# Linear attention rebuilt on channel-major r and k, halves of 64 tokens and 64x64 array tiles, ahead of a mixture of experts and a dense pair

## Chip, cores and metric

One core of one Trainium2 chip. The metric is the device time of one execution in microseconds (us). The profile follows one execution and shows five engines: PE (TensorE, with PEld for its weight loads), DVE (VectorE), ACT (ScalarE), POOL (GpSimd) and SP (SyncE, which here only issues DMAs).

## What is computed

```python
# stage 1: decaying linear attention; B=4, H=8 heads, S=768 tokens, D=48 channels
state = zeros(B, H, D, D)
for t in range(S):
    cur = einsum('bhd,bhe->bhde', u * k[t], v[t])
    y[t] = einsum('bhd,bhde->bhe', r[t], state + cur)
    state = w[:, :, None] * state + einsum('bhd,bhe->bhde', k[t], v[t])
x = y as rows of 384, one for each of the 3072 tokens
# stage 2: route every token to its best expert of 8
expert = argmax(x @ w_gate); gate = its softmax probability
x = gate * (relu(x @ w1[expert]) @ w2[expert])          # 384 -> 1024 -> 384
# stage 3: dense pair 384 -> 2048 -> 384
h = x @ w_in;  out = maximum(0.01 * h, h) @ w_out
```

All inputs are fp32.

## The kernel before

Stage 1 works in 24 units: 6 chunks of 128 tokens by 4 pairs of heads, each unit with all 4 batches. `rn`, `kn` and `vp` hold r, k and v with the 128 tokens on partitions and the two heads of a pair side by side (96 columns). In a unit:

- POOL multiplies k by u (L360), that by r (L363); DVE sums it to one number per token and head (L473, `own`); POOL multiplies v by it (L369). This is each token's own term of y.
- DVE scales r and k by powers of w (L475, L476).
- PE transposes both to channel-major (`transposes`, L721 and L723), ACT copies them out of PSUM (L653, and twice L655, once for each head with the other head's channels at zero).
- PE makes the scores k^T r of 128x128 tokens for each batch and head (L768), DVE masks them (L540), PE multiplies them with v into `ps_y` (L807).
- PE makes the unit's k^T v (L789) and r times the old state (L792); DVE adds the former to `state` and decays it (L549, L553), and adds the own term to `ps_y` into `yc` (L577).

A finished chunk is routed during the next: PE transposes its 4x3 blocks of `yc` (`tile`, L736), ACT copies them (L663), PE makes the logits (L746) and the ranks within experts (L753, L754). DVE runs 16 small steps (`routing`), ACT the exponential and the gating of rows (L669, L676), and POOL scatters the rows to their experts' places in DRAM (L384). POOL also splits the first expert's seven weight pieces into a high and a low part (`split_piece`, L133 and L137): four in chunk 1, two behind the last unit's work, one between the last two scatters. Chunks 1 to 4 stand in a hardware loop of two turns. Every engine has its own queue and order; they meet by semaphores. SP loads each unit's r, k and v with six DMAs.

Stages 2 and 3 come after a barrier. The edit changes nothing in them but the name of PSUM banks.

Of the kernel before, what the change touches and what calls it, by code (L numbers as in the profile page):

```python
# [6 lines left out]
I32 = mybir.dt.int32  # L7
# [6 lines left out]
def build_program(nc, r, k, v, w, u, moe_w_gate, moe_w1, moe_w2, moe2_w_in, moe2_w_out, out):  # L14
    P = 128
    B, H, S, DH = r.shape
    D = H * DH
    E = moe_w_gate.shape[1]
    FE = moe_w1.shape[2]
    FD = moe2_w_in.shape[1]  # L20
    C = S // P
    HP = H // 2
    W2 = 2 * DH
    N = B * S
# [7 lines left out]
    T0 = P // 2 + 1  # L32
# [17 lines left out]

    def att(a):
        return a.rearrange("b (q t) (c p) d -> c q t p b d", q=HP, p=P)

    r_v, k_v, v_v = att(r), att(k), att(v)
# [23 lines left out]
    with ctx:  # L78
# [8 lines left out]

        bank = [pb(f"bank{i}") for i in range(8)]
# [62 lines left out]
        with st1:  # L151
            rn = sb("rn", [P, HP, B, W2], stack=st1)
            kn = sb("kn", [P, HP, B, W2], stack=st1)
            vp = sb("vp", [P, HP, B, 2, W2], stack=st1)
            pr = sb("pr", [P, HP, B, W2], stack=st1)
            own = sb("own", [P, HP, B, 2], stack=st1)
            k_blk = sb("k_blk", [W2, B, 2, P], stack=st1)
            r_t = sb("r_t", [W2, 2, B, P], stack=st1)
            am = sb("am", [P, B, 2, P], stack=st1)
            state = sb("state", [W2, HP, B, W2], stack=st1)  # L160
            tab_r = sb("tab_r", [P, D], stack=st1)
            tab_k = sb("tab_k", [P, D], stack=st1)
            u_b = sb("u_b", [P, D], stack=st1)
            w_end = sb("w_end", [W2, HP, W2], stack=st1)
            yc = sb("yc", [P, 2, B, XW], stack=st1)
            x_t = sb("x_t", [P, 2, DC, P], stack=st1)
            wg = sb("wg", [P, DC, E], stack=st1)
            mask = sb("mask", [P, P], stack=st1)
            ones = sb("ones", [P, P], stack=st1)
            head = sb("head", [W2, 2], stack=st1)  # L170
            w_col = sb("w_col", [W2, 2, HP], stack=st1)
            pw = sb("pw", [W2, 2, HP, P + 2], stack=st1)
            warm = sb("warm", [W2, HP], stack=st1)
            w_128 = sb("w_128", [W2, HP], stack=st1)
            rank = sb("rank", [P, E], stack=st1)
            gate = sb("gate", [P, 2, B], stack=st1)
            tok_no = sb("tok_no", [P, 2, B], I32, stack=st1)

            mx = sb("mx", [P, B], stack=st1)
            sh = sb("sh", [P, B, E], stack=st1)  # L180
# [1080 lines left out]
```

## Time and profile before

| | |
|---|---|
| median of 3 runs | 875.04 us (869.81 to 875.75) |
| the profiled execution | 882.38 us, of it span 880.6 us |
| stage 1's units, first scores to last row | 17.27 to 203.97 us |
| granted TensorE clock, mean | 0.97 |

The profiled execution is 1.008 times the median. Times in the rows are from the start of its span. A matmul row gives how long one record takes through the array; records overlap, so their pace is read from the starts of runs of them. One fp32 product is two records (L768 has 384 for 24 units of 8 products), one transpose is one record.

### The profile page before, as it was taken

The numbers are of one execution on the slowest core, as the hardware profiler recorded it, in microseconds if no ns is written. First come the engines' busy times: TensorE is split into PE (matmuls) and PEld (weight loads), VectorE is DVE, ScalarE is ACT, GpSimd is POOL, SyncE is SP. The second block draws the span as 40 slices with busy tenths as digits, with TensorE's granted clock in tenths as the row PEclk, the third lists the DMA queues.
The fourth block names the chain that finished last, engine by engine and source line by source line (L and its number), as shares of the span: only waits on it lengthen the run. The fifth ranks groups of instructions, "written<-read, shape, count | busy, mean of one in ns | idle before, by whom it ended". The sixth has DMA issues, their size and how long they took to land.

```text
span 880.6 us, 13367 instructions
## 1 busy us (share of the span) xinstructions
PE 822.3 (93%) x4856; PEld 772.8 (88%) x4856; DVE 370.7 (42%) x711; ACT 227.2 (26%) x422; POOL 361.3 (41%) x383
## 2 busy tenths in 40 slices
PE   3999999995499999988998999999999999999996
PEld 3999899995499999988997998898998998998895
DVE  5766576865222333222226343243343343243222
ACT  1224233332111221211111323233223223223221
POOL 7684564474366778767989301001001001001001
PEclk9999799996699999999999999999999999999998
DMA  8679345421647655565444100000000000000000
GB/s 165 149 189 224 66 107 119 79 80 54 151 103 107 142 141 140 99 129 127 146 143 109 36 1 37 1 1 36 0 1 37 0 0 36 0 0 36 1 1 36
DMA packets 109523, 66.72 MB, mean 76 GB/s; under 512 B 85901, under 2 KB 103341, under 8 KB 109485
## 3 DMA queue, kind: packets, MB, share of 16 engines
q1 hardware_dynamic: 96008, 50.96, 26.1%
q10 hardware_dynamic: 10405, 5.79, 3.4%
q0 software_dynamic: 3072, 9.45, 2.8%
q8 instruction: 24, 0.39, 0.2%
q14 instruction: 14, 0.11, 0.0%
HBM read 51.62 MB, written 14.59 MB: 75 GB/s over the span
## 4 chain that ended last, share of the span: by engine, by line
PE 51%; POOL 14%; issue 5%; DMA 2%; DVE 1%; POOLq 0%; SPq 0%; ACT 0%; DVEq 0%
PE bank L1077 23%; PE bank L1056 23%; POOL w_lo L137 9%; POOL w_hi L133 4%; PE bank L1018 3%; DMA stage<-in_moe_w 2%; PE bank L1002 2%; POOL tick L123 1%; DVE x_hi L1197 0%; POOL out_rows L946 0%; DVE x_lo L1200 0%; PE bank L985 0%; POOLq L130 0%; POOLq L136 0%; SPq L897 0%
## 5 line engine op out<-in xcount | busy, mean ns | idle before, releaser
L946 POOL DMA_INDIRECT out_rows<-rows,ids_i x24 | 23.4, 974 | 359.6 <-ACT rows L1153 354.1
L1218 DVE TENSOR_TENSOR h_lo<-gf,h_hi 128x512 fp32r<-128x512 f32 x96 | 68.7, 716 | 228.3 <-ACT h_hi L1144 226.5
L137 POOL TENSOR_TENSOR w_lo<-stage,w_hi 128x768 fp32r<-128x768 f32 (+1 forms) x70 | 146.8, 2097 | 5.8
L1077 PE MATMUL bank<-w_hi,h_hi 128*128 128x384 f32 x384 | 130.4, 340 | 0.0
L1077 PE MATMUL bank<-w_lo,h_hi 128*128 128x384 f32 x384 | 129.3, 337 | 0.0
L1077 PE MATMUL bank<-w_hi,h_lo 128*128 128x384 f32 x384 | 129.1, 336 | 0.0
L1140 ACT ACTIVATE hc<-bank 128x512 f32<-128x512 f32 x96 | 57.5, 599 | 273.2 <-PE bank L1056 273.2
L1056 PE MATMUL bank<-x_hi,w_hi 128*128 128x512 f32 x288 | 114.0, 396 | 2.2 <-DVE x_lo L1200 2.2
L1056 PE MATMUL bank<-x_lo,w_hi 128*128 128x512 f32 x288 | 114.1, 396 | 0.0
L1056 PE MATMUL bank<-x_hi,w_lo 128*128 128x512 f32 x288 | 113.8, 395 | 0.0
L1182 DVE SCALAR_TENSOR_TENSOR h_lo<-bank,h_hi 128x416 fp32r<-128x416 f32 x64 | 37.9, 592 | 147.9 <-ACT h_hi L1121 147.9
L1077 PEld LDWEIGHTS bank<-w_hi,h_hi 128*128 128x128 f32 x384 | 72.1, 188 | 7.1 <-issue 3.5
L1121 ACT ACTIVATE h_hi<-bank 128x416 fp32r<-128x416 f32 x64 | 33.1, 517 | 172.7 <-PE bank L1002 172.7
L1077 PEld LDWEIGHTS bank<-w_hi,h_lo 128*128 128x128 f32 x384 | 72.2, 188 | 3.5
L133 POOL TENSOR_SCALAR w_hi<-stage 128x768 fp32r<-128x768 f32 (+1 forms) x70 | 65.2, 932 | 20.6 <-DMA stage<-in_moe_w 20.3
L1018 PE MATMUL bank<-h_hi,w_hi 128*128 128x416 f32 x192 | 67.9, 354 | 5.0 <-POOLq L143 5.0
L1077 PEld LDWEIGHTS bank<-w_lo,h_hi 128*128 128x128 f32 x384 | 72.2, 188 | 0.0
L1215 DVE SCALAR_TENSOR_TENSOR gf<-bank,hc 128x512 f32<-128x512 f32 x96 | 65.7, 684 | 12.1 <-ACT hc L1140 12.1
L1002 PE MATMUL bank<-x_hi,w_hi 128*128 128x416 f32 x192 | 67.8, 353 | 0.1
L1002 PE MATMUL bank<-x_lo,w_hi 128*128 128x416 f32 x192 | 67.5, 352 | 0.0
L1002 PE MATMUL bank<-x_hi,w_lo 128*128 128x416 f32 x192 | 67.5, 352 | 0.0
L1018 PE MATMUL bank<-h_hi,w_lo 128*128 128x416 f32 x192 | 67.2, 350 | 0.0
(148 smaller groups left out, 1387.3 us busy)
## 6 DMA issues: line engine op xcount, KB each, us to landing
stage<-in_moe_w SPq DMA_DIRECT2D x24, 512.0 KB, 5.9
stage<-in_moe_w SPq DMA_DIRECT2D x32, 384.0 KB, 3.2
rows<-x_rows ACTq DMA_DIRECT2D x9, 625.6 KB
x_rows<-pad_row SPq DMA_DIRECT2D x8, 625.6 KB
rn<-in_r SPq DMA_DIRECT2D x48, 96.0 KB, 2.6
kn<-in_k SPq DMA_DIRECT2D x48, 96.0 KB, 2.7
vp<-in_v SPq DMA_DIRECT2D x48, 96.0 KB, 2.6
stage<-in_moe_w_in SPq DMA_DIRECT2D x6, 512.0 KB, 3.9
```

The source lines that it names most:

```text
L133: eng.tensor_scalar(w_hi[:, buf, off:off + cols], stage[:, h, 0:cols], 1.0, 0.0, ALU.mult, ALU.add).then_inc(split_hi, 1)
L137: i = eng.tensor_tensor(w_lo[:, buf, off:off + cols], stage[:, h, 0:cols], w_hi[:, buf, off:off + cols].bitcast(F32), ALU.subtract)
L946: pool.indirect_dma_start(out, bass.IndirectOffsetOnAxis(ap=idx.bitcast(U32), axis=0), rows[:, t, 0:D], None).then_inc(stored, 16)
L1002: i = pe.matmul(ps_h[f % 2][:, 0:U], ww[:, b, o:o + P], x[:, b, d, 0:U], start=d == 0 and ww is w_hi and x is x_hi, stop=d == DC - 1 and x ...
L1018: i = pe.matmul(ps_y[d][:, 0:U], ww[:, b, o:o + P], h[:, f % NB, 0:U], start=f == 0 and ww is w_hi and h is h_hi, stop=f == FC - 1 and h i ...
L1056: i = pe.matmul(ps_h[f % 2][:, :], ww[:, 0, o:o + P], x[:, b, d, :], start=d == 0 and ww is w_hi and x is x_hi, stop=d == DC - 1 and x is ...
L1077: i = pe.matmul(ps_o[t][:, 0:D], x[:, f % NB, t * P:(t + 1) * P], ww[:, 1, o:o + D], start=f == 0 and x is h_hi and ww is w_hi, stop=f == ...
L1121: act.activation(h_hi[:, f % NB, 0:U], ps_h[f % 2][:, 0:U], ACT.Relu).then_inc(h_hi_ok, 1)
L1140: act.activation(hc[:, f % 2, :], ps_h[f % 2][:, :], ACT.Copy).then_inc(d_ok, 1)
L1182: dve.scalar_tensor_tensor(h_lo[:, f % NB, 0:U], ps_h[f % 2][:, 0:U], 0.0, h_hi[:, f % NB, 0:U].bitcast(F32), ALU.max, ALU.subtract).then_ ...
L1215: dve.scalar_tensor_tensor(gf[:, f % 2, :], ps_h[f % 2][:, :], 0.01, hc[:, f % 2, :], ALU.mult, ALU.max).then_inc(g_ok, 1)
L1218: dve.tensor_tensor(h_lo[:, f % NB, :], gf[:, f % 2, :], h_hi[:, f % NB, :].bitcast(F32), ALU.subtract).then_inc(gl_ok, 1)
```

## The change

- The host lays r and k out channel-major, v token-major with both heads side by side; SP loads a unit with four DMAs of 96 KB (2 KB runs) and one of 192 KB. Channels of the first head are on partitions 0 to 47, those of the second on 64 to 111; partitions between are zeroed once.
- The PE transposes of r and k, and the ACT copies of them, go. Instead PE transposes the scaled k alone to token-major (`k_rows`) and ACT copies it (`ka_copy`).
- A chunk of 128 tokens is taken as two halves of 64. Scores are made within a half only; the state is carried from half to half (`x_st`, four slots; `v_st`, the decayed copy made by ACT).
- The products address 64 rows by 64 columns of the array: scores, k^T v, r times state, and scores times v.
- The own term's sum over channels is a product with `sel` on PE (in `k_rows`) in place of the DVE reduction.
- DVE makes r*u*k in one instruction, and scales r; POOL scales k.
- `yc` has three buffers instead of two; the logits use two column halves of the array.
- All of stage 1 is written out, without loops; all seven splits of the first expert's weights lie in it.

The core of the diff (loads, dropped parts and the setup of tables left out):

```diff
             @blk.gpsimd
+                def scaled_k(g):
+                    pool.wait_ge(ruk_ok, g + 1)
+                    pool.tensor_tensor(kk, kk, pw[...], ALU.mult).then_inc(k_ok, 1)
+                def own_terms(g):
+                    pool.wait_ge(ka_out, g + 1)
+                    pool.tensor_tensor(pr[:, g % 2], v_u[:, i], a_s..., ALU.mult).then_inc(own_ok, 1)
+                scaled_k(0)
+                scaled_k(1)
+                pool.memset(tick[:, :], 0.0).then_inc(consts, 1)
+                pool.iota(...)                       # five of them, each .then_inc(consts, 1)
+                for g in range(UN):
+                    scaled_k(g + 2)
+                    own_terms(g + 1)
+                    if c >= 2 and q == 0:
+                        scatter(c - 2)
+                    if g in SPLIT_AT:                # {1: 0, 2: 1, 4: 2, 5: 3, 7: 4, 10: 5, 14: 6}
+                        split_piece(...)
             @blk.vector
+                def scale(g):
+                    dve.scalar_tensor_tensor(ruk[0:R2, g % 2], k_u[0:R2, i], u_col[0:R2, q:q + 1], r_u[0:R2, i],
+                                             ALU.mult, ALU.mult).then_inc(ruk_ok, 1)
+                    dve.tensor_tensor(rr, rr, pw[...], ALU.mult).then_inc(r_ok, 1)
+                def masks(g):
+                    dve.wait_ge(s_mm, g + 1)
+                    dve.tensor_tensor(am[:, g % 2], ps_s[...], mask_l[...], ALU.mult).then_inc(masked, 1)
+                def state(g, j):
+                    dve.wait_ge(m_mm, g + 1)
+                    dve.scalar_tensor_tensor(x_st[0:R2, q, slot(c, j + 1)], ps_m[0:R2, j, 0:B * DH], w_64[0:R2, q:q + 1],
+                                             v_st[0:R2, q], ALU.mult, ALU.add).then_inc(x_ok, 1)
+                for g in range(UN):
+                    masks(g + 1)
+                    scale(g + 2)
+                    # routing steps, if c > 0 and q >= 2
+                    state(g + 1, 0)
+                    rows_out(g)
+                    state(g + 1, 1)
             @blk.scalar
+                for g in range(UN):
+                    ka_copy(g + 1)                   # 128x448 and 128x8 out of PSUM
+                    # x_copy, exponentials
+                    decayed(g + 1, 0)
+                    # x_copy
+                    decayed(g + 1, 1)
+                    # gates
             @blk.tensor
+                def scores(g):
+                    pe.wait_ge(r_ok, g + 1)
+                    pe.wait_ge(k_ok, g + 1)
+                    for b in range(B):
+                        for j in range(2):
+                            for t in range(2):
+                                ins = pe.matmul(ps_s[halves[j], t, b * L:(b + 1) * L], k_u[heads[t], i, b, halves[j]],
+                                                r_u[heads[t], i, b, halves[j]], start=True, stop=True)
+                def k_rows(g):
+                    for b in range(B):
+                        pe.transpose(ps_x[:, b * R2:(b + 1) * R2], k_u[0:R2, i, b, :], ident[0:R2, 0:R2])
+                    for b in range(B):
+                        for j in range(2):
+                            ins = pe.matmul(ps_x[halves[j], KA + 2 * b:KA + 2 * b + 2], ruk[0:R2, g % 2, b, halves[j]],
+                                            sel[0:R2, :], start=True, stop=True)
+                def update(g):
+                    for b in range(B):
+                        for j in range(2 if c < C - 1 else 1):
+                            for t in range(2):
+                                ins = pe.matmul(ps_m[heads[t], j, b * DH:(b + 1) * DH],
+                                                km[halves[j], b, heads[t]], v_u[halves[j], i, t, b, :], ...)
+                def from_state(g):
+                    for b in range(B):
+                        for j in range(2):
+                            for t in range(2):
+                                pe.matmul(ps_y[halves[j], t, b * DH:(b + 1) * DH], r_u[heads[t], i, b, halves[j]],
+                                          x_st[heads[t], q, slot(c, j), b * DH:(b + 1) * DH], ...)
+                def within(g, other):
+                    for b in range(B):
+                        for j in range(2):
+                            t = 1 - j if other else j
+                            ins = pe.matmul(ps_y[halves[j], t, b * DH:(b + 1) * DH], am[halves[j], g % 2, t, b, :],
+                                            v_u[halves[j], i, t, b, :], ...)
                 def logits(c, b):
                     for d in range(DC):
-                        i = pe.matmul(ps_lg[:, b, :], x_t[:, b % 2, d, :], wg[:, d, :], ...)
+                        for j in range(2):
+                            ins = pe.matmul(ps_lg[halves[j], b, :], x_t[:, b, d, halves[j]], wg[:, d, :], ...)
+                pe.wait_ge(consts, CONSTS)           # 9
+                scores(0); k_rows(0); update(0)
+                for g in range(UN):
+                    scores(g + 1)
+                    # logits(c, 2 * q - 1) if 0 < q < 3
+                    k_rows(g + 1)
+                    from_state(g)
+                    within(g, False)
+                    update(g + 1)
+                    # tile(c, 2 * q) if q < 2; ranks if q == 2
+                    within(g, True)
+                    # logits(c, 2 * q), tile(c, 2 * q + 1) if q < 2
+                pe.wait_ge(y_out, UN)
+                for b, to in enumerate((ps_x, ps_s[:, 0], ps_m[:, 0], ps_s[:, 1])):
+                    tile(C, b, to)
```

## Rows read from the trace of the kernel before

**Rows 1.** The page: share of the span in which each engine is busy.
```profile
PE 822.3 (93%) x4856; PEld 772.8 (88%) x4856; DVE 370.7 (42%) x711; ACT 227.2 (26%) x422; POOL 361.3 (41%) x383
```

**Rows 2.** Stretches: length, busy PE, PEld, DVE, ACT, POOL; clock, DMA share, GB/s.
```profile
77.24:113.37 36.13, 33.82 (x266) 33.35 (x265) 19.93 (x50) 11.08 (x21) 17.97 (x22) 0.86 0.55 120
113.37:144.04 30.67, 29.37 (x267) 28.63 (x266) 23.44 (x50) 11.08 (x21) 18.06 (x22) 1.00 0.49 103
...
203.97:232.13 28.16, 7.82 (x41) 7.35 (x41) 8.41 (x51) 4.32 (x9) 10.31 (x10) 0.54 0.32 94
232.13:464.00 231.87, 226.69 (x1242) 224.08 (x1243) 65.28 (x111) 44.02 (x88) 175.43 (x172) 0.99 0.59 130
```

**Rows 3.** Timeline of PE, one unit without routing: start, duration, group, count.
```profile
25.48 1.98 PE L768 MATMUL bank<-r_t,k_blk 96*128 96x128 f32 x16
27.30 0.60 PE L721 MATMUL bank<-ident,rn 128*96 128x128 f32 x4
...
28.17 0.84 PE L789 MATMUL bank<-vp,kn 128*96 128x96 f32 x8
28.85 1.06 PE L792 MATMUL bank<-state,r_t 96*128 96x96 f32 x8
29.74 1.95 PE L807 MATMUL bank<-vp,am 128*128 128x96 f32 x16
31.53 1.98 PE L768 MATMUL bank<-r_t,k_blk 96*128 96x128 f32 x16
```

**Rows 4.** Timeline of PE behind a wait: the first two logit records together.
```profile
155.65 0.29 PE L746 MATMUL bank<-wg,x_t 128*128 128x8 f32 x2
```

**Rows 5.** The same two records by line: shortest, median, longest duration in ns.
```profile
L746 PE MATMUL bank<-wg,x_t x2: 175/216/256, 155.6 to 155.7; 128*128 128x8 f32 x2
```

**Rows 6.** DVE's groups in the units: count, busy us, mean ns, idle before.
```profile
L540 DVE TENSOR_TENSOR am<-bank,mask 128x512 f32<-128x512 f32 x48 | 31.0, 682 | 4.6 <-PE bank L768 4.5
L476 DVE TENSOR_TENSOR kn<-kn,tab_k 128x384 f32<-128x384 f32 x22 | 20.4, 926 | 0.0
...
L549 DVE TENSOR_TENSOR state<-bank,state 96x384 f32<-96x384 f32 x24 | 13.3, 554 | 34.3 <-PE bank L792 31.2 <-remote 3.1
```

**Rows 7.** DVE's group of 512 elements from two SBUF tiles, stage 3.
```profile
L1218 DVE TENSOR_TENSOR h_lo<-gf,h_hi 128x512 fp32r<-128x512 f32 x96 | 68.7, 716 | 228.3 <-ACT h_hi L1144 226.5 <-issue 1.8
```

**Rows 8.** POOL's groups in the units.
```profile
L369 POOL TENSOR_TENSOR pr<-vp,own 128x192 f32<-128x192 f32 x46 | 29.0, 651 | 15.4 <-DVE own L473 9.9 <-DMA x_rows<-yc,row_i 5.5
L363 POOL TENSOR_TENSOR pr<-pr,rn 128x384 f32<-128x384 f32 x22 | 24.4, 1110 | 1.7
...
L384 POOL DMA_INDIRECT x_rows<-yc,row_i x17 | 16.9, 996 | 10.8 <-DVE row_i L527 5.9 <-issue 4.7
```

**Rows 9.** ACT's group of 512 elements out of PSUM in the units.
```profile
L653 ACT ACTIVATE r_t<-bank 96x512 f32<-96x512 f32 x23 | 13.6, 591 | 50.5 <-PE bank L723 43.4 <-issue 7.1
```

**Rows 10.** Timeline around a split: POOL's and DVE's instructions side by side.
```profile
36.19 2.36 POOL L137 TENSOR_TENSOR w_lo<-stage,w_hi 128x1024 fp32r<-128x1024 f32 x1
36.62 2.33 DVE L553 TENSOR_TENSOR state<-state,w_end 96x384 f32<-96x384 f32 x1
```

**Rows 11.** Timeline of the start: SP's issues and POOL's first product.
```profile
0.81 0.91 SPq L266 DMA_DIRECT2D w_col<-in_w  x2
1.77 0.47 SPq L271 DMA_DIRECT2D rn<-in_r  x1
...
8.88 1.00 POOL L360 TENSOR_TENSOR pr<-kn,u_b 128x384 f32<-128x384 f32 x1 [1.60 <-DMA vp<-in_v]
```

**Rows 12.** Timeline of the tail: DVE's first routing step of the last chunk.
```profile
211.40 0.19 DVE L492 TENSOR_REDUCE mx<-bank 128x4 f32<-128x32 f32 x1 [7.42 <-PE bank L746]
```

**Rows 13.** Timeline of PE in chunk 2, where the clock falls.
```profile
91.86 0.89 PE L789 MATMUL bank<-vp,kn 128*96 128x96 f32 x8 [1.92 <-DVE yc L577]
...
94.78 3.71 PE L807 MATMUL bank<-vp,am 128*128 128x96 f32 x16
98.28 3.67 PE L768 MATMUL bank<-r_t,k_blk 96*128 96x128 f32 x16
```

More of the change, by code:

```diff
@@ L151, in build_program @@
         with st1:
[L152 to L160, printed above, removed]
@@ new lines, in _ @@
+                link(pool.memset(sel[heads[1], 1:2], 1.0))
+                link(pool.affine_select(out=mask[:, :], in_=ones[:, :], compare_op=ALU.is_gt, fill=0.0,
+                                        base=0, pattern=[[1, P]], channel_multiplier=-1))
+                for j in range(2):
+                    link(pool.tensor_copy(mask_l[halves[j], :], mask[halves[j], halves[j]]))
+                pool.memset(v_st[:, :, :], 0.0).then_inc(consts, 1)
+                pool.memset(x_st[:, :, 0, :], 0.0).then_inc(consts, 1)
@@ L405, in _ @@
-                pool.sem_inc(yc_free, 1)
-                pool.sem_inc(yc_free, 1)
-                pc = expert_pieces(0)
-                chunk(0, 0)
-                chunk(1, 1)
-                with pool.Fori(0, C // 2 - 1) as t:
-                    chunk(t * 2 + 2, 0)
-                    chunk(t * 2 + 3, 1)
-                own_terms(C - 1, HP - 1)
-                for n in range(HP, NPE - 1):
-                    split_piece(pool, n, n % 2, 0, pc[n], n in ENDS)
-                scatter(C - 2, C % 2)
@@ L598, in _ @@
-                for q in range(HP):
-                    unit(C - 1, q, (C - 1) % 2, True)
-                routing(C, (C - 1) % 2, range(1, RS + 1))
+                dve.wait_ge(rows_0, 32)
+                scale(0)
+                scale(1)
+                dve.wait_ge(consts, CONSTS)
+                masks(0)
+                state(0, 0)
+                dve.tensor_copy(rank[:, :], rank_no[:, :])
+                dve.tensor_copy(region[:, :], region_no[:, :])
+                link(dve.tensor_copy(run[:, 0, :], region_no[:, :]))
@@ L603, in _ @@
+                for b in (1, 3):
+                    dve.wait_ge(yt_mm, (C - 1) * B + (b + 1))
+                    dve.tensor_copy(x_t[:, b].rearrange("p c t -> p (c t)"), ps_s[:, b // 2, 0:D]).then_inc(yt_dve, 1)
+                routing(C, range(1, RS + 1))
                 dve.wait_ge(route, C * RS + RS)
@@ L745, in logits @@
                     for d in range(DC):
[L746 removed]
+                        for j in range(2):
+                            ins = pe.matmul(ps_lg[halves[j], b, :], x_t[:, b, d, halves[j]], wg[:, d, :],
+                                            start=d == 0, stop=d == DC - 1)
                     if b == B - 1:
[L748 removed]
+                        ins.then_inc(lg_mm, 1)
                 def ranks(c):
```

659 lines of the change are left out of this document (301 added, 358 removed).

## The prediction, made before the result was known

> **What bounds the kernel now.** I read the page first: PE is busy 93% of the span [rows 1]. An average over three stages says little, so I cut the span into stretches [rows 2]. Stages 2 and 3 (from 232.13 us) keep PE full and are not edited; what the change is worth must come out of the 232.13 us before them: start 17.27, units 186.70, tail 28.16. In the units PE is the bound: in a steady chunk of 30.67 us it is busy 29.37, DVE 23.44, POOL 18.06, ACT 11.08 [rows 2].
>
> The busy time of PE counts overlapping records, so I price by pace, from starts of successive runs [rows 3]. 16 records of L768 (128 stationary columns, 128 moving) fill 25.48 to 27.30, 0.114 us each; L807 (128 stationary, 96 moving) 0.112; L792 the same, 0.111; the transposes 0.109; L789 (96 stationary, 96 moving) 0.085. With 96 moving columns the pace still follows the stationary ones: 0.112 at 128, 0.085 at 96, so 0.00084 a column. A unit is 16 x 0.114 + 8 x 0.109 + 8 x 0.085 + 8 x 0.111 + 16 x 0.112 = 6.05 us, which is the distance of the two L768 runs. Routing of a chunk adds 12 transposes, 24 logit records and 4 rank records: 12 x 0.109 + 28 x 0.112 = 4.4. A chunk is then 28.6, and the steady one takes 30.67: 2.1 of waits, some 0.5 a unit. Chunk 2 takes 36.13 because the clock fell (mean 0.86).
>
> **The new work of PE, in records.** Scores 32 (64 stationary columns), transposes of k 4 (128), sums with `sel` 16 (64), `update` 32 (48 stationary), `from_state` 32 (64), `within` 32 (64): 148 where there were 56. The rows fix the price only from both sides.
>
> - *One after another.* Continuing the line of the two paces, 64 stationary columns cost 0.058 and 48 cost 0.045. Then a unit is 32 x 0.058 x 3 + 32 x 0.045 + 4 x 0.11 + 16 x 0.058 = 8.4 us: PE loses 2.3 us a unit.
> - *Side by side.* If different corners of the array load and multiply at once, what is left is the distance at which PE can start records. The smallest that the trace shows: two logit records take 0.29 together while the second takes 0.256, so they start 0.03 apart [rows 4, 5]. At 0.03 the four array-tile products cost 128 x 0.03 = 3.84. The `sel` sums use all rows and split the array only by columns; the trace has nothing like it, I take the middle, 0.044: 0.7. With the transposes 0.45: 5.0.
>
> I take side by side: in every product except `update` two neighbours lie in different row halves, and 0.03 is a distance seen in this trace, though only between two records whose weights could be loaded during a wait. That is the weakest step here. A change between 64-wide and full use of the array may have to empty it; the trace has none. The bounds are nothing and the part of a record that overlap hides now, 0.275 - 0.112 = 0.16; I take 0.08 for each of 5 changes a unit, 0.4. So a unit is 5.4. Routing: 12 transposes 1.3, 48 half-width logit records x 0.044 = 2.1, ranks 0.45, changes of mode 0.4: 4.3 a chunk. With the old 2.1 of waits a chunk is 4 x 5.4 + 4.3 + 2.1 = 28.0.
>
> The Trainium skill has a rule on each side. TensorEngine Tiling (Array Packing), section Performance Considerations, gives each matmul some 60 cycles whatever its columns, which is an estimated 0.025 us at 2.4 GHz and near the 0.03 of the rows. The Trainium skill's page TensorE: Matmul & The Clock Gate, section "Wait — 56ns, not 53.3ns?", has a case in which firmware decodes each matmul at some 62 ns; by that 148 records would be an estimated 9.2 us and the change a loss. No row here has such short records in a long run, so it is open which holds.
>
> **The other engines' new work per unit.** DVE: the r*u*k and the r product are 512 elements from two SBUF tiles, 0.716 each when POOL is quiet [rows 7]; the 384-element L476 takes 0.926 next to POOL [rows 6], so up to 1.2 each: 1.4 to 2.4, taken 2.0. One mask of 512 instead of two, 0.68. Two state steps of 192 elements, each above half of L549's 0.554 and below it: taken 0.35, 0.7. Row output 0.55, as L549. Routing: some 0.9 (16 short steps over four units). Sum 4.8. POOL: `scaled_k` 512/384 x 1.11 = 1.5, `own_terms` two times 0.65 = 1.3 [rows 8], scatter four times 1.0 a chunk, and seven splits of about 3: 2.8 + 1 + 0.9 = 4.7. ACT: the copy of 448 elements about 0.6 [rows 9], small ones, two decays, routing: under 3. All below 5.4 to 7, so hidden as long as PE needs that; what a quick PE would meet is below.
>
> The new waits: `scores(g + 1)` stands first in PE's order and waits for r_ok and k_ok. Behind it everything of PE is queued. The ring is scores (1.0 and 0.15 to the end), masks 0.68, r*u*k 1.0, `scaled_k` 1.5, and four hand-overs that I put at 0.1: 4.7 us a unit, less than PE's own. POOL's splits stand in this ring's path and hold DVE's two-input instructions: the decay of the state, 384 elements, took 2.33 beside a split of 2.36 [rows 10]. A split begins after `own_terms`, and at 7 us a unit it is over before the next r*u*k is asked for. At cost nothing go: the three ACT copies and the DVE reduction (their engines were idle behind PE), the loads (five DMAs instead of six a unit, ahead of use), the third `yc` buffer (it only removes a wait for scatters), and the program's greater length, unless fetching it stalls PE.
>
> **Start and tail.** SP issues six small loads at about 0.45 and then ten of 0.5 up to unit 1's k and r, with two DMAs of zeros between [rows 11]: 0.8 + 2.7 + 2.5 + 1.0 + 2.0 = 9.0, landing at some 12. PE waits for nine constants, which POOL makes behind `scaled_k(1)`: 12 + 0.8 + 1.4 + 0.6 = 14.8, against 17.27. Gain 2.4. The bounds are 0 and 4.5 (if only unit 0 were waited for). In the tail the last row is out at 203.97 and the first routing step starts at 211.40 [rows 12], 7.4 later; four transposes into four banks, copies by two engines and 48 records of logits at the low clock make it about 5: gain 2.5, bounds 1 and 4. The rest of the 28.16 (routing, slot tables, last scatters, barrier, first loads) stays.
>
> **The sum.** Chunk 0, without routing: 4 x 5.5 and 2 for the low clock of the start, 24. Five chunks of 28.0, less 0.5 for the halved `update` of the last chunk times four units: 138. Together 162 against 186.7: 24.7 less; chunk 2's fall of the clock (5.5 us over a steady chunk) is part of that. With 2.4 and 2.5 it is 29.6. From 882.4 that gives 852.8 in the profiled execution, and divided by 1.008, 846 for the median. The largest unknown, the mode changes, moves this by 0.4 x 24 = 10 either way; the pace of `sel` sums and logits between 0.03 and 0.058 by about 9: 825 to 866 for this case.
>
> **The rivals.**
>
> *Slower: the 64-wide products don't overlap.* Unit 8.4 + 0.4, routing 12 x 0.109 + 48 x 0.058 + 0.45 + 0.4 = 4.9; chunk 4 x 8.8 + 4.9 + 2.1 = 42.2; together 38 + 211 - 3 = 246, 59 more than before, less 4.9: +54, 929. It decides from a mean pace of 0.038 us for the 128 tile records of a unit (where PE's new sum passes the old). For it: 2.6 times the records, and every long run in the trace keeps at least 0.085. Against: the trace's pace follows the width of the weights, and neighbours here use different rows. A mean near 0.04 would leave the time where it is. (The 62 ns of the Trainium skill's page TensorE: Matmul & The Clock Gate, same section, would end in this rival, an estimated 0.8 us a unit later still.)
>
> *PE out of the way.* If tiles start closer than 0.03, DVE, POOL and the ring of 4.7 us bound: with splits and scatters in POOL's order about 5.6 a unit, 24 x 5.6 + 2 = 136, 51 less, with start and tail 56 less: 820. For it: 4 corners at once would need only a quarter of 0.058.
>
> *The clock.* It fell in chunk 2 some 1.3 us after PE had waited 1.92, and L807 went from 0.112 to 0.219 a record [rows 13]. If small tiles with short waits keep the granted clock at its lower level, 1.2 GHz, for half of the units, PE adds some 5 a unit there, 60 in all, against the 30 gained: 905. For it: PE waits more where others catch up; against: most of the time PE stays the busiest.
>
> **Chances.** Forecast 0.45; PE out of the way 0.2; no overlap 0.2; low clock or overlap that is only partial, from 866 to 905, 0.15. The range for 8 in 10 goes from 815 to 915. A measurement of this kernel can't tell less than 1% from nothing. Faster by over 1% (below 866): 0.68; within 1% (866 to 884): 0.07; slower by over 1%: 0.25.
>
> **What will show it.** Starts of successive records of scores and `within`: 0.03 apart (forecast), near 0.058 (no overlap), under 0.02 (PE out of the way). Distance of two units' score runs: 5.5 without routing, 7 with. First scores at 14.8. The granted clock of the units near 0.95. DVE's mask waits for PE, not PE for k_ok. Wrong would make me: firmware-like pace of records, stalls of PE's fetch, mode changes that cost more than 0.16, or splits that hold the ring.

## The result, and the profile after

The changed kernel takes 885.45 us (883.44 to 886.74, 4 runs) where the kernel before takes 874.76 (869.81 to 875.75, 4 runs): ratio 1.013, 95% interval 1.009 to 1.018. It is slower by a little over 1%, where 846 was forecast. Medians here and below are of all executions, ratios only of those within 1.5% of their kernel's fastest. Its profiled execution took 883.44, with a span of 881.7.

The page, those lines of it that answer to [rows 1], and those in 40 slices that show the finding at once:

```profile
PE 816.5 (93%) x7136; PEld 752.5 (85%) x7136; DVE 336.8 (38%) x659; ACT 214.6 (24%) x435; POOL 334.3 (38%) x330
...
PEclk9875566555599999999999999999999999999999
```

PE's share is what it was, so the first line says nothing. The second does: a slice is 22 us, and from the fourth to the eleventh the granted clock is 0.5 to 0.6. The stretches, as in [rows 2] (length, busy PE, PEld, DVE, ACT, POOL; clock, DMA share, GB/s). From the row at 71.10 on, three rows hold four units each; the one before them holds three, the one behind them the last five:

```profile
0.00:18.28 18.28, 0.00 (x0) 0.00 (x0) 6.16 (x25) 1.50 (x3) 7.55 (x24) 1.00 0.60 134
18.28:47.94 29.66, 26.91 (x673) 24.69 (x673) 16.05 (x32) 6.70 (x18) 17.51 (x13) 0.85 0.78 205
47.94:71.10 23.16, 21.59 (x517) 18.88 (x515) 13.15 (x25) 6.65 (x18) 13.40 (x10) 0.72 0.78 230
71.10:105.68 34.58, 33.42 (x663) 29.48 (x661) 17.84 (x41) 9.62 (x25) 19.14 (x16) 0.50 0.49 142
105.68:139.65 33.97, 30.98 (x661) 27.30 (x660) 17.14 (x41) 9.62 (x25) 16.45 (x15) 0.60 0.35 107
139.65:173.47 33.82, 31.04 (x663) 27.19 (x661) 17.14 (x41) 9.62 (x25) 13.98 (x13) 0.60 0.32 96
173.47:211.45 37.98, 36.20 (x664) 32.28 (x662) 15.19 (x44) 9.13 (x22) 12.29 (x11) 0.50 0.07 23
211.45:239.90 28.45, 6.85 (x70) 6.13 (x69) 10.62 (x58) 3.34 (x7) 7.75 (x8) 0.50 0.33 97
239.90:881.70 641.80, 629.49 (x3264) 586.53 (x3264) 223.53 (x353) 158.41 (x292) 226.20 (x222) 0.99 0.22 59
```

Start 18.28 (before 17.27). The units, up to the end of their last row of y, end at 212.36, 0.91 behind the cut between two rows above: 194.1 us (186.7), and the tail is 27.5 (28.16) [rows 2]. So the units lost 7.4 us where 24.7 were to be won. The steady chunk went from 30.67 to some 33.9, and DVE's work in it fell from 23.44 to 17.14, as intended; PE alone sets its length. The last stretch runs the same code as before, in 641.8 us against 648.5; over the profiles of this study it took between 641 and 655. That is in part why the two profiled spans lie 1.1 apart and the medians 10.7.

The clock of 0.85 in the second row is too high. The profile shows 1.00 until the first change of level that it recorded, here at 35.4; the four transposes at 19.35 take 0.93 us to the next start and those at 35.77 take 0.53, so the first 17 us of the units ran at the lower level too. From 18.28 to 212.36 the level was full for 27.3 us alone.

Now PE's timeline of a unit without routing, to be read against [rows 3]; here the granted clock is at its lower level, 1.2 GHz:

```profile
71.26 1.13 PE L703 MATMUL ps_s<-r_u,k_u 48*64 48x64 f32 x30
72.32 1.01 PE L719 MATMUL ps_x<-ident,k_u 112*128 112x112 f32 x4
73.26 1.02 PE L723 MATMUL ps_x<-sel,ruk 112*64 112x2 f32 x16
74.21 1.11 PE L751 MATMUL ps_y<-x_st,r_u 48*64 48x48 f32 x32
...
75.87 0.94 PE L737 MATMUL ps_m<-v_u,km 64*48 64x48 f32 x29
76.59 0.94 PE L766 MATMUL ps_y<-v_u,am 64*64 64x48 f32 x13
77.24 0.37 PE L703 MATMUL ps_s<-r_u,k_u 48*64 48x64 f32 x2
```

There is no idle time in it, and it takes 77.24 - 71.10 = 6.14 us. The old unit took 6.05 at full clock. One run of 32 records at the full level, and how long a single record of it takes (shortest, median, longest in ns):

```profile
36.87 0.68 PE L751 MATMUL ps_y<-x_st,r_u 48*64 48x48 f32 x32
```
```profile
L751 PE MATMUL ps_y<-x_st,r_u x32: 218/218/253, 36.9 to 37.3; 48*64 48x48 f32 x32
```

The last of 32 starts 0.68 - 0.218 = 0.46 behind the first, so the records follow each other at 0.015 us. At the lower level the same 32 go from 74.21 to 75.10, 0.028 each. The four corners do work side by side, at half the distance that I had forecast; and the clock takes that factor of two away again.

### The profile page after: what moved, and what is told of

The parts are those of the page before. It is cut to its first block, busy times and chain, and to the rows that moved or that the text cites. A ratio compares the mean times of both kernels' runs of the same rounds, so it can differ in the third digit from the quotient of the medians.

```text
span 881.7 us, 17577 instructions
## 1 busy us (share of the span) xinstructions
PE 816.5 (93%) x7136; PEld 752.5 (85%) x7136; DVE 336.8 (38%) x659; ACT 214.6 (24%) x435; POOL 334.3 (38%) x330
## 4 chain that ended last, share of the span: by engine, by line
PE 70%; DVE 1%; DMA 1%; POOL 0%; ACTq 0%; issue 0%; ACT 0%; DVEq 0%
PE bank L1072 23%; PE bank L1051 22%; PE bank L997 12%; PE bank L1013 12%; PE bank L980 1%; DMA rows<-x_rows 1%; DVE x_hi L1192 1%; POOL out_rows L941 0%; DVE x_lo L1195 0%; ACTq L899 0%; DVE h_lo L1213 0%; ACT h_hi L1116 0%; ACTq L1104 0%; ACTq L1095 0%; DVE h_lo L1177 0%
## 5 line engine op out<-in xcount | busy, mean ns | idle before, releaser
L1213 DVE TENSOR_TENSOR h_lo<-gf,h_hi 128x512 fp32r<-128x512 f32 x96 | 71.8, 748 | 225.7 <-ACT h_hi L1139 223.8
L359 POOL TENSOR_TENSOR k_u<-k_u,pw 112x512 f32<-112x512 f32 x24 | 40.5, 1686 | 84.7 <-DVE ruk L449 84.7
```

The source lines that it names most:

```text
L359: pool.tensor_tensor(kk, kk, pw[0:R2, 1, q, 2:L + 2].unsqueeze(1).broadcast_to([R2, 2 * B, L]), ALU.mult).then_inc(k_ok, 1)
L1213: dve.tensor_tensor(h_lo[:, f % NB, :], gf[:, f % 2, :], h_hi[:, f % NB, :].bitcast(F32), ALU.subtract).then_inc(gl_ok, 1)
```

## The experiments

Each of them is told as its edit to the changed kernel, unless it says otherwise. "Clock" is the mean granted TensorE clock of the span of a profiled run; stages 2 and 3, where it is 0.99, make up most of that span, so small differences in it are large ones in the units. PE's full clock is 2.4 GHz.

An execution's time also holds stages 2 and 3, which the edits leave alone and which vary by 14 us, and the runs were made on different chips. So this table splits each profiled execution (one per kernel; us). The units go from the first scores to the end of the last row of y; "full" is the time of them that the trace records at the full level.

| kernel | units | of them full | stages 2 and 3 |
|---|---|---|---|
| before | 186.7 | 168.6 | 648.5 |
| before, unrolled | 180.2 | 172.4 | 643.6 |
| changed | 194.1 | 27.3 | 641.8 |
| one corner after another | 285.1 | 0 | 640.7 |
| four added products | 186.1 | 119.5 | 643.2 |
| two added products | 204.9 | 44.4 | 654.1 |
| scatters moved | 191.1 | 27.3 | 647.3 |
| one scatter a unit | 179.3 | 34.1 | 649.3 |
| zeroing late | 195.4 | 13.7 | 643.3 |
| combination with two products | 196.7 | 37.5 | 654.6 |
| tables early | 184.7 | 27.3 | 645.5 |
| tables early, 32 products first | 185.7 | 34.5 | 641.3 |
| three edits | 177.2 | 122.9 | 643.8 |
| four edits | 174.6 | 133.1 | 650.0 |

### Unrolling alone

The kernel before, with its loops over chunk pairs written out in all five programs, nothing else:

```
-                with pe.Fori(0, C // 2 - 1) as t:
+                for t in range(C // 2 - 1):
```

> The kernel before with stage 1 written out, nothing else. If writing out is what costs (PE waits for its own instructions, then the clock falls), this run shows issue gaps on PE of 1 us and more and loses 5 us or more against before. If it is only together with the dense small products that it costs, this run is like before within 1%, perhaps 2 to 4 us faster, since chunk 2's gap at the loop's turn goes.

872.44 us against 871.65 for the kernel before on the same chip: 1.001 (0.996 to 1.007). A steady chunk of it:

```profile
104.00:134.70 30.70, 29.68 (x269) 28.97 (x268) 24.01 (x52) 11.14 (x22) 18.48 (x22) 1.00 0.51 108
```

30.70 against 30.67 [rows 2], at full clock. Unrolled code by itself costs nothing with these records: 269 in 30.7 us here, 661 in 34 in the changed kernel. In the profiled execution the clock did not fall in chunk 2, and the units took 180.2 us; the 186.7 of the kernel before hold that fall.

### One corner after another

In the four products by corners the loop over batches goes innermost, so that four successive products, eight records, lie in the same corner:

```
-                    for b in range(B):
-                        for j in range(2):
-                            for t in range(2):
+                    for j in range(2):
+                        for t in range(2):
+                            for b in range(B):
```

> The kernel after, with the four batches innermost in scores, update, from_state and within, so that successive records address the same 64x64 corner; same products, same number. If the overlap of corners is real, these records go from 0.027 apart at the low clock (mean) to about 0.1 at low and 0.055 at high clock, and a unit gets 2 to 5 us longer: 50 to 100 us in all. If corners never overlapped, nothing changes.

973.13 us, one run: 88 us slower than the changed kernel, and its units 91 longer; one without routing takes 9.57 (24.69 to 34.26). PE's timeline:

```profile
24.95 2.31 PE L703 MATMUL ps_s<-r_u,k_u 48*64 48x64 f32 x30
27.19 1.01 PE L719 MATMUL ps_x<-ident,k_u 112*128 112x112 f32 x4
28.13 1.02 PE L723 MATMUL ps_x<-sel,ruk 112*64 112x2 f32 x16
```

30 records in 27.19 - 24.95 = 2.24, 0.075 each, where the changed kernel shows 0.035 for this line at the same clock (71.26 to 72.32). So the overlap between corners is real and worth most of those 88 us (the changed kernel also had the full level for 27 us). The four transposes give the level away: 0.94 us from 27.19 to 28.13, as in the row at 72.32; at full clock they take 0.53 (next experiment). PE is at the lower level. Between the starts of two records it had no gap of 1 us before 122 us, and that one is a wait for ACT. Late instructions are thus not needed for a low clock.

### Large products against the low clock

Four, or two, products of 128x128 on constants in each unit ahead of its scores, whose result the scores overwrite; they add work and leave none out. The wait for the mask of the unit before (`masked`) moves ahead of them:

```
+                    for n in range(4):
+                        pe.matmul(ps_s[:, 0, 0:P], ident[:, :], ones[:, :], start=True, stop=True)
                     pe.wait_ge(r_ok, g + 1)
                     pe.wait_ge(k_ok, g + 1)
```

> The kernel after, with four extra full 128x128 fp32 products (8 records, 0.9 us at the high clock, 1.8 us at the low one) ahead of each unit's scores; their result is overwritten. If the low clock is what ate the gain and small tiles are too little work to bring it back, the granted clock in the units rises from 0.61 to above 0.85, units without routing take about 5 us instead of 6.14, and the run is 10 to 30 us faster than after in spite of the added work. If the clock is not the cause (ring of DVE and POOL, or issue gaps), the units get longer by 0.9 to 1.8 us, 20 to 40 us slower than after.

> Two extra full products (4 records) a unit instead of four. If it is the full-array work that lifts the clock, in proportion, the clock of the units lies between after (0.61) and four extra products (0.83 or so), and the time within 5 us of that run: less added work against a lower clock. If four only lifted it by chance, the clock here is as in after and the run 5 to 20 us slower than after.

With four: 890.81 us (1.017, 1.009 to 1.025), clock 0.941 instead of 0.896. With two: 909.31 (1.043, 1.035 to 1.051), clock 0.902. Neither is faster than the changed kernel (1.013), so on the time both expectations failed; units of 4.7 us and a clock that follows the dose came as expected. The profile with four is of the fastest of its runs, 878.68; the clock of the others was 0.907 to 0.930. A unit of it, at full clock:

```profile
174.17 0.69 PE L705 MATMUL ps_s<-r_u,k_u 48*64 48x64 f32 x32
174.80 0.60 PE L721 MATMUL ps_x<-ident,k_u 112*128 112x112 f32 x4
175.33 0.63 PE L725 MATMUL ps_x<-sel,ruk 112*64 112x2 f32 x16
...
177.78 1.16 PE L699 MATMUL ps_s<-ones,ident 128*128 128x128 f32 x8
```

From the scores to the added products PE needs 177.78 - 174.17 = 3.61 us for what took 6.14 above. (This unit, one of the last, has only half of `update`. It makes no difference: one with the whole of it, from 72.45 to 77.17, takes 4.72 with its added products, this one 4.69; and at the lower level the changed kernel takes 6.14 for either.) That is the price of the clock: 2.5 us in each unit without routing. The added products cost 1.1 a unit at full clock, 26 in all, and bring the full level for part of the time: 119.5 us of the units against 27.3. With two it is 44.4, and their cost outweighs it. Of the 24 us by which its profiled execution is slower than the changed kernel's, 11 lie in the units and 12 in stages 2 and 3, so only the 11 can be put down to the products.

### The instructions that come late

The second thing in the changed kernel's trace. In its units PE waited 9.5 us on "issue", in those of before 1.1. PE's weight loads, the time that they waited in the units (us in total, times, longest):

```profile
PEld ps_l L781 <- issue: 5.2, 9, 1.1
PEld ps_s L703 <- issue: 5.0, 14, 0.5
```

"Issue" is waiting for nothing that the profile shows; I read it as PE's next instruction not being there yet. Early on these are single gaps of 1.2 to 1.8 us (here and below from the start of one record to the start of the next; the rows show the idle part), at 37.7, 44.3 and 57.6; later they come bunched, and the timeline of POOL and PE together shows beside what:

```profile
119.08 0.96 POOL L381 DMA_INDIRECT x_rows<-yc,row_i  x1 [0.30 <-issue]
...
119.85 0.34 PE L703 MATMUL ps_s<-r_u,k_u 48*64 48x64 f32 x4 [0.41 <-issue]
...
120.61 0.40 PE L703 MATMUL ps_s<-r_u,k_u 48*64 48x64 f32 x3 [0.42 <-issue]
...
121.61 0.96 POOL L381 DMA_INDIRECT x_rows<-yc,row_i  x1 [0.30 <-issue]
122.04 0.32 PEld L781 LDWEIGHTS ps_l<-wg,x_t 128*64 128x64 f32 x4 [0.52 <-issue]
```

While POOL starts its four scatters, PE gets two to four records at a time, then waits 0.4 to 0.6. Three runs on this. In the first the scatters of the first two chunks come at units 13 and 18 and the others at the end (with a fourth `yc` buffer); in the second each unit issues one scatter instead of the chunk's first issuing four; in the third the zeroing of `x_rows` goes from units 0 to 7 to units 13 to 20 (in this order):

```
-                    if c >= 2 and q == 0:
-                        scatter(c - 2)
+                    if g == 13:
+                        scatter(0)
+                    if g == 18:
+                        scatter(1)
```
```
-                    if c >= 2 and q == 0:
-                        scatter(c - 2)
+                    if c >= 2:
+                        scatter(c - 2, [q])
```
```
-                    if g < E:
-                        zero_rows(g)
+                    if 13 <= g < 13 + E:
+                        zero_rows(g - 13)
```

> The kernel after with four yc buffers, scatters of chunk 0 and 1 at units 13 and 18 and the other four behind the last unit, instead of at units 8, 12, 16, 20. If POOL's indirect DMAs are what makes PE's instructions trickle (gaps of 0.5 to 0.7 us between records at 88, 120, 154 and 190 us), the long units 9, 13, 17 and 21 (11 to 13 us) shrink to about 9 and only one or two near 14 and 19 are long: the units together 8 to 14 us shorter, the tail 10 to 12 longer. If the gaps come from somewhere else, they stay where they are.

> The kernel after with one scatter of 128 rows in each of the four units of a chunk, not four in a row in its first. If POOL's indirect DMAs slow PE's instructions only while several are under way, the gaps of 0.5 to 0.7 us go and the run gains 8 to 15 us on after. If each such DMA costs PE its 3 to 4 us / 4 wherever it stands, the gaps appear in every unit and the time stays within 3 us of after.

> The kernel after with the eight writes of zero rows (626 KB each) at units 13 to 20 instead of 0 to 7. If the early gaps of 1.2 to 1.8 us at 38, 44 and 58 us are instructions that come late because these DMAs fill the queues (DMA share 0.78 there), they go, and similar ones appear about units 13 to 20. If PE's fetch is late by itself whenever the clock is high, they stay.

*Moved:* 887.51 us, one run, no gain. The bunched gaps moved with the scatters:

```profile
125.06 0.96 POOL L381 DMA_INDIRECT x_rows<-yc,row_i  x1 [0.30 <-issue]
125.10 0.30 PE L783 MATMUL ps_l<-wg,x_t 128*64 128x8 f32 x3 [0.44 <-issue]
...
126.33 0.96 POOL L381 DMA_INDIRECT x_rows<-yc,row_i  x1 [0.30 <-issue]
127.37 0.16 PE L725 MATMUL ps_x<-sel,ruk 112*64 112x2 f32 x1 [0.34 <-issue]
```

They now stand at about 124 to 128 and 168 to 171, and nowhere at the old places. The units became 3 us shorter and not the 8 to 14 of the expectation. So the bunched gaps belong to the row of indirect DMAs.

*One a unit:* median 875.55 (857.29 to 885.19, 10 runs) against 876.56 for the kernel before on that chip, equal to it and about 10 us below the changed kernel. Its runs scatter widely. The ratio of 0.985 (0.979 to 0.992) rests on the three fastest of the ten, so I go by the medians here; the run with the tables early, which holds this edit too, agrees with them (0.9996, 12 runs). No row of gaps stands beside the single scatters. Its stretches:

```profile
96.10:120.60 24.50, 22.48 (x657) 19.98 (x656) 18.29 (x42) 9.73 (x25) 16.21 (x14) 0.86 0.50 140
120.60:197.10 76.50, 74.39 (x1477) 66.27 (x1476) 36.81 (x96) 20.88 (x53) 33.85 (x30) 0.53 0.23 70
```

The first is a chunk at clock 0.86: 24.5 us, the shortest of any kernel so far, before's 30.67 included. In the second, at 0.53, chunks take 32.8: PE waits for hardly anything and is slow. The level fell at 125.5, at the end of a wait for DVE; nothing was late there:

```profile
125.48 0.64 PE L789 MATMUL ps_l<-oh,mask 128*128 128x32 f32 x2 [1.14 <-DVE oh L515]
```

*Zeroing late:* 886.25, one run, no gain. The gaps at 44.3 and 57.6 are gone, but in place of the one at 37.7 stands a longer one:

```profile
39.35 0.69 PE L703 MATMUL ps_s<-r_u,k_u 48*64 48x64 f32 x32 [2.35 <-issue]
```

This can't be put down to the zeroing. The run with one scatter a unit, which issues the zero rows where the changed kernel does, has the same picture up to 60 us:

```profile
39.40 0.69 PE L703 MATMUL ps_s<-r_u,k_u 48*64 48x64 f32 x32 [2.35 <-issue]
```

The run with the scatters moved, also with early zeroing, has its early gaps at 35.9, 43.6 and 64.0. So where they fall differs between kernels whose edits start only behind unit 7, and one profile of each can't show what moves them.

### The combination with two products

Two added products, one scatter a unit, zeroing late, and on DVE the r*u*k of unit g + 2 ahead of the masks of unit g + 1:

```
+                    if g + 2 < UN:
+                        scale(g + 2)
                     if g + 1 < UN:
                         masks(g + 1)
-                    if g + 2 < UN:
-                        scale(g + 2)
```

> The kernel after with two extra full products a unit, scatters spread, zero rows late, and on DVE the scaling for unit g+2 ahead of the mask of g+1. If clock and gaps are the two costs, this is the fastest of these: clock in the units above 0.8, units without routing about 4.3 us, the run 15 to 35 us faster than after and 5 to 20 faster than before. If something else bounds, it stays near after.

897.44 us (1.023, 1.017 to 1.030), a miss. In the profiled executions its units are only 2.6 us longer than the changed kernel's, its stages 2 and 3 12.8. Two stretches of it:

```profile
55.10:90.50 35.40, 33.94 (x1029) 29.90 (x1028) 27.08 (x55) 14.19 (x37) 25.59 (x20) 1.00 0.51 148
...
129.10:166.30 37.20, 37.20 (x673) 33.21 (x672) 15.87 (x41) 9.68 (x26) 16.69 (x15) 0.50 0.53 156
```

The first row is six units in 35.4 us, 5.9 each with routing and ballast, at full clock. Then came one gap of 1.62 us at 92.55, the clock fell at 93.2 and did not come back in the units; PE was busy without a break (37.20 of 37.20) at the lower level. A PE that never waits does not get its clock back by that.

### The start, and a warm array

The first edit is this, on top of one scatter a unit; the second run adds to it 32 products of 128x128 on constants ahead of `scores(0)`, behind a wait for `ident` alone.

```
-                scaled_k(0)
-                scaled_k(1)
                 pool.memset(tick[:, :], 0.0).then_inc(consts, 1)
                 pool.iota(slot_no[:, :], [[1, LOOKS]], base=0, channel_multiplier=0).then_inc(consts, 1)
...
                 pool.iota(tok_no[:, :, :], [[P, 3], [S, B]], base=-3 * P, channel_multiplier=1).then_inc(consts, 1)
+                scaled_k(0)
+                scaled_k(1)
```

> The changed kernel with two shifts on GpSimd and nothing else: the scatter DMAs one per unit, as in the run before, and the tick and the five index tables, for whose last one TensorE waits before its first product, ahead of the two first k products instead of behind them. Theory (the start is held by that wait alone): first scores at about 15.4 us instead of 18.28, where the first scaled k is done at 15.3, and the time some 2 us below that of the spread scatters alone, 873, if the low clock of the units stays as it is. Rival (the second scaled k, done at 17.7, holds the second scores, and the 3 us come back as a wait of TensorE in the first units): no change, 875.

> As the run with the early tables, and 32 full 128x128 products on constants before the first scores, while TensorE has nothing else to do; their result is overwritten. If the low clock is only a starting condition, from which the units can't climb because they wait too little or too shortly, the granted clock is at its full level from the first scores on and stays there, units without routing take 4.4 to 5.7 us, and the time is 835 to 850. If the units' own records bring the clock down (the theory that I hold), it starts full, falls within the first chunks and stays mostly low: clock of the span 0.90 to 0.92, time within 5 us of the run without the products.

*Tables early:* 872.35 us (866.09 to 879.25, 12 runs), ratio 0.9996 (0.997 to 1.002), clock 0.902. The first scores start behind `scaled_k(0)`, 2.8 us sooner:

```profile
15.48 1.13 PE L703 MATMUL ps_s<-r_u,k_u 48*64 48x64 f32 x32 [15.48 <-POOL k_u L359]
```

Of the 2.8 us, 0.47 come back as PE's wait ahead of the second scores, put down to the load of `wg` and not to the second scaled k. The time lies within the 2 us by which theory and rival differed, so it doesn't tell them apart.

*With 32 products before them:* 869.71 (863.01 to 880.20, 12 runs), ratio 0.996 (0.992 to 0.9994), clock 0.892.

```profile
2.20 9.01 PE L794 MATMUL ps_s<-ones,ident 128*128 128x128 f32 x64 [2.20 <-POOL ident L343]
15.40 0.83 PE L703 MATMUL ps_s<-r_u,k_u 48*64 48x64 f32 x32 [4.19 <-POOL k_u L359]
16.17 1.01 PE L719 MATMUL ps_x<-ident,k_u 112*128 112x112 f32 x4
```

The products were over after 9 us, PE idled 4.19, the scores still began at the faster pace, and the transposes behind them are slow (0.94 us): the clock fell at 15.8. So the warm start was lost in the wait, and this doesn't test a unit chain that begins warm. What it does show is later: four times the level came back, at 46.5, 63.6, 111.4 and 159.2, and each time it fell again within 14 us. The low level is no leftover of the start.

### Four products again, with the scatters spread

The tables early, one scatter a unit and four added products; and the same with the zeroing late.

> As the run with the early tables, and four full 128x128 products in every unit before its scores, as in the run with four products, where the scatters still came four at a time. There the granted clock was 0.941 and stretches of late instructions at the scatters each ended in a fall. Theory (a gap of issue is what lets the clock fall once the ballast is in): without the bunched scatters the clock stays full for most of the units, 0.96 or more for the span, units without routing 4.7, a chunk some 26 to 28 us, and the time 835 to 855, faster than both kernels. Rival (the level is set by the small products, the ballast lifts it only in part, as two products a unit did): clock 0.92 to 0.94, time 880 to 890.

> The last run (spread scatters, early tables, four 128x128 products in every unit) with the zeroing of the rows in memory, eight DMAs of 626 KB, moved from units 0 to 7 to units 13 to 20. In the last run two stretches with late instructions, 3.4 us at 51.8 and 1.2 at 77.6 of the span, fall in the units that issue these DMAs or just behind, and the clock fell at 55.6. Theory (the fetch of TensorE's instructions shares the DMA engines with that traffic, and each late stretch costs itself and the low clock behind it): no late stretch above 1 us before unit 13, clock full up to there, 0.97 for the span, time 845 to 858. Rival (the late stretches come wherever the traffic is, or from the program's length): they turn up in units 13 to 20 instead or stay, and the time stays at 860 to 868.

*Three edits:* 864.15 us (856.18 to 870.43, 6 runs), ratio 0.989 (0.984 to 0.993), clock 0.955: faster than the kernel before by 1.1%, than the changed one by some 2.4%. The fair comparison is with the run with the tables early, on the same chip and without the four products: 872.35, 0.9996 (0.997 to 1.002). So the products gain 8 us once the scatters are spread. The theory (835 to 855) and the rival (880 to 890) both missed. Two of its stretches:

```profile
106.90:134.00 27.10, 24.02 (x690) 21.38 (x689) 17.81 (x43) 9.72 (x25) 16.58 (x15) 1.00 0.48 134
...
161.30:191.90 30.60, 29.37 (x681) 26.45 (x680) 14.50 (x39) 8.66 (x21) 13.31 (x12) 0.78 0.10 35
```

Full clock and no bunched gaps: 27.1 us for a chunk, with 4.3 of added products in it, against 33.9 in the changed kernel. The gain is lost in part early on, where a gap of 3.4 us at 51.8 is followed by the fall at 55.6, and three units take 32.6 us.

*Four edits:* 868.63 (857.85 to 877.62, 6 runs), ratio 0.983 (0.974 to 0.991), clock 0.963. The two can't be told apart: their intervals overlap. The theory asked for 845 to 858 and no gap above 1 us before unit 13. The profile has one there:

```profile
53.42 0.24 PE L739 MATMUL ps_m<-v_u,km 64*48 64x48 f32 x2 [1.31 <-issue]
```

It is shorter than the 3.4. Others come at 107.0 (1.54) and 148.4 (2.5), in the units to which the zeroing moved, which would fit the rival; but by the two runs above such gaps move without it, so this shows no cause either.

## Why the prediction was wrong

It was wrong in its sign: 885.45, within the range and in the 0.25 that I left for slower, not in the 0.68 for faster. Point by point:

- *Side by side, 0.03 a record, "the weakest step":* the overlap is there, and the run with one corner after another costs 88 us without it. At full clock the distance is 0.015, so of the two the rival "PE out of the way" had the pace right, down to its quarter of 0.058. My 0.03, from two logit records [rows 4, 5], met the 0.028 of the lower level by chance. The 60 cycles a matmul of the Trainium skill, page TensorEngine Tiling (Array Packing), section Performance Considerations, an estimated 0.025 us at 2.4 GHz, do not hold between corners; the trace's 0.015 decides. Nor did the 62 ns of the Trainium skill's page TensorE: Matmul & The Clock Gate, section "Wait — 56ns, not 53.3ns?", show: by them the 148 records of a unit would take an estimated 9.2 us.
- *The mode changes, 0.4 a unit:* the whole unit takes 3.61 at full clock where I had 5.4, with the changes in it. They can't be large. With the halved distance this is a unit 1.8 us shorter than forecast, 43 in all.
- *"The granted clock of the units near 0.95":* this is the step that failed. The level was full for 27.3 of 194.1 us, the steady chunks at 0.50 to 0.60. By it a unit costs 6.14 instead of 3.61, some 61 us over 24 units, and a chunk without bunched gaps 32.8 (the run with one scatter a unit) against my 28.0. My slow pace of 5.4 had counted part of it already. What was left, 0.74 a unit or 18 us, and 1.8 us a chunk on the routing (32.8 - 4 x 6.14 = 8.2, where I had 6.4 with the waits), another 9, ate the gain of 24.7. I had the low clock as a rival, with 5 us a unit on top of 5.4 and half of the units low; it was 2.5 a unit on top of 3.61 and nearly all of them, so that its 60 us came out right by luck, and its chance of 0.15 was too small. Its reason was not right either: I expected it where PE waits. In 71.10 to 105.68 PE is busy 33.42 of 34.58 us at 0.50, so my argument against it, that PE stays the busiest, does not hold. The Trainium skill, page TensorE: Matmul & The Clock Gate, section Part 1: The HAM clock gate, says that the throttled level is the default and that activity releases it. The trace agrees that the units begin at the lower level (0.93 us for the first four transposes); it also shows that a PE busy by the profile can go without the release.
- *The range:* that 885.45 lies in it is luck. A unit 1.8 us cheaper than forecast and a clock that adds 2.5 nearly cancel.
- *The program's length, "at cost nothing ... unless fetching it stalls PE":* it does stall PE. The bunched gaps beside the scatters are worth about 10 us (885 to 875 when spread), the early ones 1.2 to 1.8 us each. I had named the condition and not priced it. That it is the fetch that is late is my reading; the profile shows only that PE waited for nothing that it records.
- *Start, 14.8:* it was 18.28. Two terms of my sum: SP's issues of unit 1's k and r took 1.75 and 2.00 instead of 0.5 each, so that r*u*k of unit 1 started at 14.80, not 12; from there 1.06, 1.77 and 0.58 (the tables, for the last of which PE waits) lead to 18.2:

```profile
7.54 1.75 SPq L289 DMA_DIRECT2D k_u<-in_k  x1
9.33 2.00 SPq L290 DMA_DIRECT2D r_u<-in_r  x1
...
14.80 1.06 DVE L449 SCALAR_TENSOR_TENSOR ruk<-k_u,u_col,r_u 112x512 f32<-112x512 f32 x1 [0.44 <-DMA r_u<-in_r]
...
15.94 1.77 POOL L359 TENSOR_TENSOR k_u<-k_u,pw 112x512 f32<-112x512 f32 x1 [0.63 <-DVE ruk L449]
...
18.28 0.38 PE L703 MATMUL ps_s<-r_u,k_u 48*64 48x64 f32 x3 [18.28 <-POOL tok_no L393]
```

- *Tail, a gain of 2.5:* 0.6. The last row's step ends at 212.36 and the first routing step starts at 219.20, 6.8 later against 7.4 [rows 12], all at the lower level:

```profile
219.20 0.19 DVE L504 TENSOR_REDUCE mx<-ps_l 128x4 f32<-128x32 f32 x1 [3.37 <-PE ps_l L781]
```

- *The other engines:* right at the lower level. DVE's work of a chunk fell to 17.14 us, and POOL, ACT and the ring stay below PE's 33.9. At the full level PE does wait for them now and then: in the run with one scatter a unit 1.05 us for ACT and 1.14 for DVE within 17 us.

The account of the units, an estimate from the distances of successive score runs. Take each unit at its distance at the lower level and without gaps (6.14 without routing; with it 9.08, 9.67 and 7.90), and the first two and the last as they stand: 191.4, where 162 was forecast. So the low clock alone makes the units longer than the 186.7 of before. The four units with scatters are 1.8, 3.3, 3.1 and 1.3 longer than that, 9.5 in all, and the three early gaps add 4.3. That makes 205.2; measured are 194.1, and the 11 between them are what 27.3 us at the full level gave back.

What stays open is what brings the clock down and back. In the changed kernel the falls at 38.8 and 59.3 follow single gaps of 1.3 and 1.8 us, those at 120.7 and 154.9 the bunched gaps, each of 0.4 to 0.6; in other runs they follow waits for ACT or DVE. But some such gaps have no fall behind them (1.2 to 1.3 us at 103.5, 117.1 and 130.5 with three edits), the level also comes back with no event that I can name, and the one-corner kernel was low with no gap before it. Added full-array products raise the time at the full level, four a unit far more than two; no run isolates what it is about them that does it, or puts the added products into the corners. Why PE's instructions are late beside an indirect DMA is open too; that they are is shown by moving it.

## What to carry to other kernels

Price a change that makes TensorE's work smaller at both levels of its clock: dividing full-array products into corners saves records' time, and what is saved can be lost by the clock alone; look at the granted clock of the stretch before the busy share. When a change multiplies an engine's instructions, its supply becomes a resource: look for "issue" beside GpSimd's indirect DMAs, and issue these one at a time. If the lower level can't be avoided otherwise, full-size products that nothing reads can pay for themselves. Here four a unit, 1.1 us in a unit of 3.6, gained 8 us once the scatters were spread (864 against 872) and nothing before (891 against 885); two a unit lost.

## What the runs showed of the hardware that I had not expected

- Records of different corners (L751) start 6 to 7 ns apart in groups of four, and the groups 58 ns apart at full clock, 107 at the lower level; the scores of the one-corner run average 75 ns at the lower level.
- TensorE stayed at the lower level for tens of microseconds with hardly any idle time: 54.6 us from 59.3 in the changed kernel, and all of the 37.20 above.
- Before its first recorded change the clock shows as 1.00 whatever it is: the stretch before the first scores says 1.00, and so does the whole stage 1 of the one-corner run, whose transposes (0.94 us for four, against 0.53) say that it is at the lower level. The pace of a known record is the better witness.
- Sums of two moving columns are no cheaper than their fixed distance: 16 records of L723 take 0.95 us at the lower level (73.26 to 74.21) and 0.56 at the full one, 0.035 each where I had 0.044.
